# Turning later tiles' scaled keys on VectorE in 32 by 32 blocks instead of on TensorE

## What is computed

```
for t in range(S):
    state = alpha[:, :, t, :, None] * state + np.einsum('bhd,bhe->bhde', k[:, :, t], v[:, :, t])
    y[:, :, t] = np.einsum('bhd,bhde->bhe', q[:, :, t], state)
...
    h = x @ w_in
    relu6 = np.clip(h + 3.0, 0.0, 6.0)
    g = h * relu6 / 6.0
    return (g @ w_out)
...
    h = x @ w_in
    r = np.maximum(h, 0.0)
    g = r * r
    return (g @ w_out)
```

## Time and profile before

| | |
|---|---|
| median of 3 runs | 888.85 us (888.41 to 888.9) |
| the profiled execution | 888.96 us, span 887.2 us |
| PE busy | 879.8 us, 99% of the span |
| PEld busy | 726.7 us |
| DVE busy | 352.5 us |
| ACT busy | 373.0 us |
| POOL busy | 314.3 us |

### The profile page before, as it was taken

The page is one execution under the profiler, slowest core; times in us unless marked ns, Lnnn a source line. Parts: engine busy times, 40 slices in busy tenths (PEclk is TensorE's granted clock), DMA queues, the critical chain, the costliest instruction groups (busy, mean ns, idle before and its releaser), DMA issues.

```text
span 887.2 us, 12951 instructions
## 1 busy us (share of the span) xinstructions
PE 879.8 (99%) x5032; PEld 726.7 (82%) x5032; DVE 352.5 (40%) x581; ACT 373.0 (42%) x722; POOL 314.3 (35%) x249
## 2 busy tenths in 40 slices
PE   8999999999999999999999999999999999999998
PEld 7888888888888888878888888888888888888886
DVE  8786456456546554663133331221211211211211
ACT  4765354445534543444344533433332433433322
POOL 2655343334324333342332333333232333323232
PEclk9999999999999999999999999999999999999999
DMA  9621111212211111210122100000000000000001
GB/s 354 243 90 59 55 54 54 72 37 77 84 55 46 63 55 53 68 56 9 36 93 93 64 1 0 36 1 1 37 0 1 36 1 0 36 1 1 36 0 37
DMA packets 19966, 46.51 MB, mean 52 GB/s; under 512 B 3264, under 2 KB 7104, under 8 KB 19904
## 3 DMA queue, kind: packets, MB, share of 16 engines
q1 hardware_dynamic: 19904, 45.68, 14.9%
HBM read 38.98 MB, written 4.72 MB: 49 GB/s over the span
## 4 chain that ended last, share of the span: by engine, by line
PE 97%; DMA 1%; ACT 0%; SPq 0%; issue 0%; ACTq 0%
PE h_ps L924 45%; PE o_ps L937 44%; PE att_ps L834 2%; PE att_ps L879 2%; DMA w_in_raw<-w_in 1%; PE att_ps L844 1%; PE att_ps L895 1%; PE att_ps L855 1%; SPq L329 0%; PE h_ps L866 0%; ACT k_tok L477 0%; PE att_ps L820 0%; PE att_ps L866 0%; SPq L335 0%; SPq L331 0%
## 5 line engine op out<-in xcount | busy, mean ns | idle before, releaser
L438 POOL TENSOR_TENSOR g_parts<-h_act,g_parts 128x512 fp32r<-128x512 f32 x192 | 256.4, 1335 | 550.9 <-ACT g_parts L528 550.9
L937 PE MATMUL o_ps<-g_parts,w_out_hi 128*128 128x512 f32 x1152 | 327.0, 389 | 0.0
L924 PE MATMUL h_ps<-x_parts,w_in_hi 128*128 128x512 f32 x1152 | 297.8, 394 | 0.0
L937 PEld LDWEIGHTS o_ps<-g_parts,w_out_hi 128*128 128x128 f32 x1152 | 216.2, 188 | 45.0
L924 PEld LDWEIGHTS h_ps<-x_parts,w_in_hi 128*128 128x128 f32 x1152 | 213.0, 188 | 45.3 <-issue 0.4
L528 ACT ACTIVATE g_parts<-h_act 128x512 fp32r<-128x512 f32 x192 | 121.3, 632 | 268.6 <-PE o_ps L937 225.9
L714 DVE SCALAR_TENSOR_TENSOR h_act<-h_ps,h_gate 128x512 f32<-128x512 f32 x96 | 66.4, 691 | 290.5 <-ACT h_gate L523 290.5
L937 PE MATMUL o_ps<-g_parts,w_out_lo 128*128 128x512 f32 x576 | 165.6, 389 | 0.0
L924 PE MATMUL h_ps<-x_parts,w_in_lo 128*128 128x512 f32 x576 | 161.8, 389 | 0.0
L924 PEld LDWEIGHTS h_ps<-x_parts,w_in_lo 128*128 128x128 f32 x576 | 108.1, 188 | 22.7
L937 PEld LDWEIGHTS o_ps<-g_parts,w_out_lo 128*128 128x128 f32 x576 | 108.1, 188 | 22.4
(11 more groups left out here) (116 smaller groups left out, 465.9 us busy)
## 6 DMA issues: line engine op xcount, KB each, us to landing
inputs<-att_in SPq DMA_DIRECT2D x20, 770.0 KB, 4.6
w_in_raw<-w_in SPq DMA_DIRECT2D x8, 768.0 KB, 8.2
w_out_raw<-w_out SPq DMA_DIRECT2D x8, 768.0 KB, 8.8
inputs<-v_in SPq DMA_DIRECT2D x20, 288.0 KB, 3.0
result<-inputs SPq DMA_DIRECT2D x18, 256.0 KB, 2.4
x_parts<-tails SPq DMA_DIRECT2D x120, 16.0 KB, 1.8
x_mid<-att_in SPq DMA_DIRECT2D x2, 770.0 KB, 8.9
first_v<-v_first SPq DMA_DIRECT2D x4, 384.0 KB, 10.0
```

The source lines that it names most:

```text
L438: nc.gpsimd.tensor_tensor(g_parts[:, g % 2, 1, :], h_act[:, g % 2, :], g_parts[:, g % 2, 0, :].bitcast(F32), ALU.subtract).then_inc(g_lo, 1)
L924: last = nc.tensor.matmul(h_ps[g % 2][:, :], w[:, m, cols], x_parts[:, n % 2, part, m, :], start=m == 0 and i == 0, stop=m == KT - 1 and i ...
L937: return nc.tensor.matmul(o_ps[m][:, :], w[:, f, m * P:(m + 1) * P], g_parts[:, g % 2, part, :], start=f == 0 and w is w_out_hi and part = ...
```

## The change

For tiles 4 to 19 the four transposes on TensorE and the copy on ScalarE are left out. VectorE takes their place: a new `turn_keys` on its queue makes 16 transposes a tile, each of a block of 32 features by 32 tokens for the four pairs at once (32 partitions by 128 columns). Eight stand in the step before the tile is scored, at the end of that step's work, and eight in the step of its scoring, ahead of `mask_later`. `k_tok` becomes two places that take turns: a tile of its own and, for odd tiles, a part of `x_mid` that is not yet in use. `add_up` waits for the new semaphore `keys_turned`, and so does the load of the tile that takes over the input slot. Tiles 0 to 3 keep their transposes and copies. Some single-column helpers (`ones`, `in_range`) move into other tiles, to make room.

```diff
         def k_tok(t):
+            return pairs(x_mid[:, KT - 1, (NBLK - 2) * BLK:(NBLK - 1) * BLK]) if t > BATCH and t % 2 else first_k_tok[:, :, :]
...
                     sp.wait_ge(y_made, t - 1)
+                    past(sp, keys_turned, BLOCKS * BLOCKS * (t - 1 - BATCH) if t - 2 < TILES - BATCH else 0)
...
                 for t in tiles_at(g, 1):
                     x_high(t)
-                    if t < TILES - BATCH:
-                        copy_keys(t)
...
+            def turn_keys(t, tokens):
+
+                dve.wait_ge(k_scaled, t + 1)
+                dve.wait_ge(u_made, max(t - 1, BATCH))
+                scaled = pairs(slot(t)[:, 0:PAIRS * TILE])
+                for b in tokens:
+                    for a in range(BLOCKS):
+                        nc.vector.transpose(k_tok(t)[b * BLOCK:(b + 1) * BLOCK, :, a * BLOCK:(a + 1) * BLOCK],
+                                            scaled[a * BLOCK:(a + 1) * BLOCK, :, b * BLOCK:(b + 1) * BLOCK]).then_inc(keys_turned, 1)
...
+                for t in tiles_at(g, -1):
+                    if t < TILES - BATCH:
+                        turn_keys(t, range(0, BLOCKS // 2))
                 for t in tiles_at(g, 0):
+                    if t < TILES - BATCH:
+                        turn_keys(t, range(BLOCKS // 2, BLOCKS))
                     mask_later(t)
...
             def score_late(t):
-                pe.wait_ge(k_back_copied, min(t, TILES - BATCH))
+                if t == BATCH:
+                    pe.wait_ge(k_back_copied, BATCH)
...
             def add_up(t):
-                pe.wait_ge(k_back_copied, t + 1)
+                if t < BATCH:
+                    pe.wait_ge(k_back_copied, t + 1)
+                else:
+                    pe.wait_ge(keys_turned, BLOCKS * BLOCKS * (t - BATCH + 1))
...
                 for t in tiles_at(g, 1):
-                    if t < TILES - BATCH:
-                        turn_keys(t)
                     attend(t)
```

More of the change, by code:

```diff
@@ L59 @@
 FIRST_SCORE_AT = (3, 6, 9, 12)
+BLOCK = 32
+BLOCKS = P // BLOCK
 DECAYS_LEAD = 3
@@ L148, in chunked_program @@
         masked_t = sb("masked_t", [P, 2, PAIRS, TILE])
-        k_tok = sb("k_tok", [P, PAIRS, ROWS])
+        first_k_tok = sb("first_k_tok", [P, PAIRS, P])
         state = sb("state", [ROWS, BATCH, PAIRS, HD])
@@ L155, in chunked_program @@
         ranges = sb("ranges", [ROWS, 2, TILES])
-        in_range = sb("in_range", [ROWS, 2 * TILES])
-        in_range_all = sb("in_range_all", [ROWS, 1])
-        ones = sb("ones", [ROWS, 1])
         x_flat = x_mid[:, :, :].rearrange("p a b -> p (a b)")
         causal_odd = x_mid[:, KT - 1, NBLK * BLK - TILE:]
+        in_range = masked_t[0:ROWS, 0, 0, 0:2 * TILES]
+        in_range_all = masked_t[0:ROWS, 0, 0, 2 * TILES:2 * TILES + 1]
         out_stage = inputs[:, 0, 0:KT * BLK].rearrange("p (a b) -> p a b", a=KT)
@@ L217, in permuted_values, with k_tok @@
             return inputs[:, t % 2, SLOT_W + DM + j * HD:SLOT_W + DM + (j + 1) * HD]
+        def k_tok(t):
+            return pairs(x_mid[:, KT - 1, (NBLK - 2) * BLK:(NBLK - 1) * BLK]) if t > BATCH and t % 2 else first_k_tok[:, :, :]
         def outputs(t, half):
@@ L278, in chunked_program @@
         masked = sem("masked")
+        keys_turned = sem("keys_turned")
         k_back = sem("k_back")
@@ L476, in copy_keys @@
                 past(act, u_made, t)
-                nc.scalar.activation(k_tok[:, :, :], banks(t)[2][:, 0:PAIRS * ROWS].rearrange("p (a b) -> p a b", a=PAIRS),
+                nc.scalar.activation(k_tok(t)[:, :, 0:ROWS], banks(t)[2][:, 0:PAIRS * ROWS].rearrange("p (a b) -> p a b", a=PAIRS),
                                      ACT.Copy).then_inc(k_back_copied, 1)
@@ L552, in _ @@
             act.wait_ge(init_vec, 1)
-            nc.scalar.activation(squares[:, 0:1], ones[:, :], ACT.Copy).then_inc(act_warm, 1)
+            nc.scalar.activation(squares[:, 1:2], squares[:, 0:1], ACT.Copy).then_inc(act_warm, 1)
             act.wait_ge(act_warm, 1)
@@ L738, in judge_ranges @@
                 dve.wait_ge(range_checked, 2 * TILES)
-                nc.vector.tensor_scalar(in_range[:, :], ranges[:, :, :].rearrange("p a b -> p (a b)"), RANGE_MAX, None,
+                nc.vector.tensor_scalar(in_range, ranges[:, :, :].rearrange("p a b -> p (a b)"), RANGE_MAX, None,
                                         ALU.is_le).then_inc(range_judged, 1)
                 dve.wait_ge(range_judged, 1)
-                nc.vector.tensor_reduce(in_range_all[:, :], in_range[:, :], mybir.AxisListType.X, ALU.min).then_inc(range_judged, 1)
+                nc.vector.tensor_reduce(in_range_all, in_range, mybir.AxisListType.X, ALU.min).then_inc(range_judged, 1)
             def publish_ranges():
@@ L749, in _ @@
             for m in range(KT):
-                nc.vector.memset(in_range[:, m:m + 1], 0.0).then_inc(o_free[m], 1)
-            nc.vector.memset(in_range_all[:, :], 0.0).then_inc(g_free, 2)
-            nc.vector.memset(ones[:, :], 1.0).then_inc(init_vec, 1)
+                nc.vector.memset(ranges[:, 0, m:m + 1], 0.0).then_inc(o_free[m], 1)
+            nc.vector.memset(ranges[:, 1, 0:1], 0.0).then_inc(g_free, 2)
+            nc.vector.memset(squares[:, 0:1], 1.0).then_inc(init_vec, 1)
             dve.wait_ge(init_vec, 1)
@@ L849, in turn_keys @@
                 bank_k = banks(t)[2]
-                if t >= BATCH:
-                    pe.wait_ge(masked, masks_of(t))
-                elif t >= 2:
+                if t >= 2:
                     pe.wait_ge(state_made, 2 * (t - 1))
@@ L894, in add_up @@
                             v = first_values(t)[:, 1, :, half, HD:HALF]
-                        last = nc.tensor.matmul(sums(t, half)[:, j, :], k_tok[:, j, half_rows(half)], v, start=True, stop=True)
+                        last = nc.tensor.matmul(sums(t, half)[:, j, :], k_tok(t)[:, j, half_rows(half)], v, start=True, stop=True)
                 last.then_inc(u_made, 1)
@@ L1000, in _ @@
                     pe.wait_ge(range_judged, 2)
-                    nc.tensor.matmul(att_ps[0][0:1, 0:1], in_range_all[:, :], ones[:, :], start=True, stop=True).then_inc(range_counted, 1)
+                    nc.tensor.matmul(att_ps[0][0:1, 0:1], in_range_all, causal[0:ROWS, TILE - 1:TILE], start=True, stop=True).then_inc(range_counted, 1)
 def recurrent_program(nc, block, semaphores, raw, out, out_stored, stores_issued, flags):
```

## The result

The changed kernel takes 908.32 us (906.72 to 909.09, 4 runs) against 888.68 us; the ratio is 1.0219, with a 95% interval from 1.0201 to 1.0236. It is slower by 19.6 us. The profiled execution took 908.76 us, its span is 906.9.

A forecast was written before the change was run, and what follows sets the result against it. TensorE, busy for 99% of the span, was taken to bound the kernel. 888.96 us plus 12.3 us of waits in tiles 4 to 7, less 6.26 us saved on TensorE, gave 895.0 us; range 887.5 to 901.

The forecast's parts named there:

- These twelve tiles I cost at nothing, up to about p = 0.36: Tiles 8 to 19: transposes hidden in VectorE's idle 2.74 and 1.88 us, masks some 0.6 us late against 2.7 us lead.
- p: Start-to-start time of one block transpose on VectorE: 0.31 us, bounds 0.21 and 0.365.
- a loop from masks to masks: VectorE and ScalarE without TensorE: 13.36 + 16p us from tile 4 to 5 against TensorE's 15.28, then 14.18 + 16p against 15.64.
- if tiles 8 to 19 wait too: One of the signs named for the prediction being wrong; it expected TensorE to wait for masks in tiles 4 to 7 only.
- The price of a transpose: On VectorE: 0.296 us from a line between the reciprocal and `place_state`, plus a 0.015 gap, as source partitions change: 0.31.
- Tiles 4 to 7: Weight splits fill VectorE's gaps here, so TensorE waits 2.2, 3.0, 3.5 and 3.5 us, 64p - 7.56 = 12.3 us.
- The clock: Rival, chance 0.04: TensorE's clock falls to 1.2 GHz behind each of four waits, four times 4 us more, 911 us.
- 0.39 us a tile on TensorE: `attend` starts sooner after `project` without the four transposes; sixteen tiles save 6.26 us, 882.7 us if nothing else moved.
- that tiles 4 to 7 wait, each between 2 and 3.5 us: Expected in the profile after: TensorE waits on VectorE's masks at `attend` in these tiles, all before some 105 us.
- `add_up` and the slot's load never waiting for `keys_turned`: Both new waits were left at nothing: transposes end a tile ahead of `add_up`, and the load waits for `y_made` anyway.
- p falling by the overlap where partitions stay the same: VectorE instructions on the same partitions overlap, 0.21 us start to start; rival that transposes do too: 888.6 us, chance 0.15.

The follow-up runs named there:

- filled kernel: The changed kernel with nine extra matmuls of the identity on TensorE ahead of `attend` in tiles 4 to 7: 906.31 us, run again 906.20 us.
- one source's partitions: The changed kernel with all 256 transposes reading the same 32 features, partitions 0 to 31: 890.66 us, ratio 1.0022.

## Why the prediction was wrong

The sign was right and the size was not: forecast 895.0 with a range from 887.5 to 901, measured 908.3.

**The step that failed** is "These twelve tiles I cost at nothing, up to about p = 0.36". It held the transposes of one tile against the idle time in one pass of VectorE's queue and against the lead of the masks, and found both large enough. But I had just walked a loop from masks to masks for tiles 4 to 7, and never closed the same one for tiles 8 to 19. There it is 16.64 us at p = 0.333 against TensorE's 15.64, so the lead with which a block begins is used up by its second tile. Idle time ahead of two instructions is no measure of what fits in: the 2.74 us of the earlier trace rows were there because VectorE waited for a `gate` whose time TensorE set; as soon as the transposes fill it, `x_low` and the next activation, which wait for ScalarE, follow later too. Forecast for these tiles: -4.7 us. In the filled kernel, whose clock was full, their lag grows from 13.3 to 17.3 us: +4.0. The runs with tiles 8 to 19 alone (+4.3 over before) and with one source's partitions (no such wait) show it. That is 8.7 of the 13.3 us that were missing. The last sign of being wrong that the prediction named, "if tiles 8 to 19 wait too", is what the trace shows.

The unclosed loop is not all of the 8.7, by an estimate from the same rows. At the forecast's p = 0.31, and with `place_state` at 0.73 us, the loop is 16.0 us: longer than 15.64, so the limit of p = 0.36 was wrong (it is 0.29), but short enough that the nine tiles would only have lost their saving. The 0.023 us that each transpose took beyond the forecast add 9 x 16 x 0.023 = 3.3 us, and the 0.25 us of `place_state` beside GpSimd, which the forecast did not have either, add 2.3. About 3 us are left for the loop alone. Because the loop was taken to be short, the other two seemed to cost nothing here.

**The price of a transpose**: 0.31 forecast, 0.333 measured. The row it was taken from and the reason were right, as the run with one source's partitions shows; times 64, in tiles 4 to 7, it is 1.5 us more.

**Tiles 4 to 7**: 12.3 us of waits were forecast, less 1.6 saved, 10.7; the lag at tile 7 is 13.1. The price explains 1.5. Another 1.0 came in at tile 5, where a weight split that took 1.76 us before took 2.77. The split and GpSimd's `low` beside it, before and then in the changed kernel:

```profile
51.49 1.76 DVE L729 TENSOR_TENSOR w_in_lo<-w_in_raw,w_in_hi 128x1536 fp32r<-128x1536 f32 x1
51.51 2.89 POOL L438 TENSOR_TENSOR g_parts<-h_act,g_parts 128x512 fp32r<-128x512 f32 x1 [0.65 <-ACT g_parts L528]
...
56.26 2.77 DVE L745 TENSOR_TENSOR w_in_lo<-w_in_raw,w_in_hi 128x1536 fp32r<-128x1536 f32 x1
56.13 1.29 POOL L446 TENSOR_TENSOR g_parts<-h_act,g_parts 128x512 fp32r<-128x512 f32 x1 [0.49 <-ACT g_parts L536]
```

Whichever of the two started first had its usual time (1.76 and 1.29 us), and the other was stretched. In the run with the second eight behind the masks the split starts first again, by 0.07 us, and has 1.76. That it is the meeting was not tried by itself. Tile by tile the added lag is above the forecast by 0.0, 1.8, 0.3 and 0.3 us, so the parts of 1.5 and 1.0 hold for the sum and not for each tile.

**The clock** was named as a rival at 911 us with 0.04. The fall did come, in each of the changed kernel's executions, but in its two traces at three of the four waits, and at far less than the four times 4 us: where VectorE's loop is the longer one, a slower TensorE costs nothing. It is worth next to nothing to 2.8 us.

Sum: 895.0 + 8.7 + 1.5 + 1.0 = 906.2 us, to be held against 906.2 of the filled kernel at full clock and 905.9 of the two profiled executions without the clock's part; with the 2.8 us of the first of them, 909.0, where it took 908.8.

**What held**: 0.39 us a tile on TensorE (882.7 forecast for it alone, 882.71 measured); that tiles 4 to 7 wait, each between 2 and 3.5 us; `add_up` and the slot's load never waiting for `keys_turned`; p falling by the overlap where partitions stay the same. (16 x 0.39 is 6.24 and not 6.26 us, which changes nothing.)

## What to carry to other kernels

Work that is moved onto an engine with idle time has to be put into every loop that passes through that engine, not only into the gap beside which it lands: add up the loop from one instance of the late step to the next and hold it against the stretch of the engine that bounds the kernel. If a loop is just too long, look for the place in it where the engine waits for another; work put there is free, while the same work ahead of the step that all wait for is paid in full (908 against 889.6 us for the same sixteen transposes, with the meetings with GpSimd and the clock's fall that came with them). Moved work also shifts what runs beside what: look again at the instructions whose own time has changed. And on VectorE, count short instructions from start to start, with what their partitions do from one to the next.

## What was unexpected of the hardware

A transpose of 32 partitions by 128 columns of float32 lasts 0.303 us and starts 0.334 after the last one if its source's partitions change, but 0.26 and 0.193 if neither source nor target changes them: the change costs 0.14 us an instruction. An instruction of VectorE with both inputs in SBUF that started beside a running one of GpSimd took longer: 2.77 us instead of 1.76, and 0.99 for two instead of 0.73. And equal executions of a kernel whose clock falls spread over 2.4 us (906.72 to 909.09) and 7 us (903.23 to 910.26 with tiles 4 to 7 alone, where 4.9 us of the profiled execution go back to a wait and a fall before step 0), where those without long waits spread over 0.2 to 0.9.
